# A second router written out phase by phase, and lookup tables with the columns innermost

## The reference, cut to what matters

```python
cap = N // E                       # 384
logits = x @ w_gate                # 3072 x 8
for idx in np.argsort(-logits.flatten()):
    tok, e = int(idx) // E, int(idx) % E
    if assigned[tok] >= 0 or counts[e] >= cap:
        continue
    assigned[tok] = e
    counts[e] += 1
for e in range(E):
    mask = assigned == e
    out[mask] = np.maximum(x[mask] @ w1[e], 0.0) @ w2[e]
```

## Time and profile before

| | us |
|---|---|
| median of 3 runs | 1102.71 |
| lowest, highest | 1101.93, 1104.84 |
| the profiled execution | 1102.15 |
| its span in the profile | 1100.1 |

### The profile page before, as it was taken

One profiled execution on the slowest core, in us unless ns is written; L12 is line 12 of the kernel. 1 busy time (PEld: TensorE's weight loads), 2 busy tenths in 40 slices (PEclk: granted clock), 3 DMA queues, 4 the chain that ended last, 5 costly groups with the idle time before them and its releaser, 6 DMA issues.

```text
span 1100.1 us, 22403 instructions
## 1 busy us (share of the span) xinstructions
PE 939.4 (85%) x6254; PEld 799.3 (73%) x6255; DVE 725.5 (66%) x1921; ACT 411.9 (37%) x885; POOL 189.9 (17%) x246
## 2 busy tenths in 40 slices
PE   7999999985599999999999973444379999999994
PEld 4888888874478888888888852333269898898984
DVE  5888888868865877868868685555735454555421
ACT  3555665545443452543534430000024343433410
POOL 1222222200111211111111110000021223312211
PEclk8999999998699999999999996555579999999997
DMA  9566666442161524515425150000034445354200
GB/s 217 128 145 143 141 146 145 96 154 108 54 243 38 191 63 176 191 48 199 139 100 183 48 191 31 0 0 0 1 90 151 166 150 210 123 185 156 89 29 29
DMA packets 146020, 129.13 MB, mean 117 GB/s; under 512 B 101936, under 2 KB 114224, under 8 KB 145840
## 3 DMA queue, kind: packets, MB, share of 16 engines
q1 hardware_dynamic: 137168, 99.67, 30.3%
q0 software_dynamic: 8800, 28.84, 7.7%
HBM read 107.78 MB, written 20.71 MB: 117 GB/s over the span
## 4 chain that ended last, share of the span: by engine, by line
PE 61%; DVE 17%; issue 9%; DVEq 5%; DMA 2%; ACTq 1%; ACT 1%; SPq 0%; POOL 0%; POOLq 0%
PE ps_o L1212 10%; PE ps_o L1585 8%; PE ps_s L1189 8%; PE ps_s L1569 6%; PE ps_pT L1569 6%; DVE product L1412 5%; PE ps_o L489 4%; PE ps_s L1585 4%; PE ps_t L1747 3%; PE ps_pT L470 3%; PE ps_s L457 3%; DVE arena_p L664 2%; PE ps_pT L1200 1%; DVEq L671 1%; DVEq L1415 1%
## 5 line engine op out<-in xcount | busy, mean ns | idle before, releaser
L1212 PE MATMUL ps_o<-w_split_parts,hs 128*128 x696 | 168.2, 398 | 10.7 <-ACT hs L1289 9.6
L1189 PE MATMUL ps_s<-w_split_parts,xs 128*128 x696 | 167.2, 396 | 1.5 <-ACT xs L1281 0.9
L1212 PEld LDWEIGHTS ps_o<-w_split_parts,hs 128*128 128x128 f32 x696 | 130.0, 190 | 38.6 <-issue 12.0
L1412 DVE SCALAR_TENSOR_TENSOR product<-y_sb,wg_all 128x512 bf16<-128x512 f32 x232 | 150.8, 687 | 6.8 <-ACT y_sb L1307 1.8
L1189 PEld LDWEIGHTS ps_s<-w_split_parts,xs 128*128 128x128 f32 x696 | 129.7, 190 | 28.0 <-issue 2.4
L773 ACT ACTIVATE arena_p<-arena_p,min_s 128x256 f32<-128x256 f32 (+1 forms) x192 | 91.7, 484 | 12.0 <-DVE min_s L653 10.9
L1585 PE MATMUL ps_o<-w_split_parts,hs 128*128 128x512 f32 x384 | 94.7, 398 | 0.0
L1403 DVE TENSOR_TENSOR w_split_parts<-raw,w_split_parts 128x1024 f32 (+1 forms) x68 | 78.7, 1220 | 5.9 <-ACT w_split_parts L1300 4.5
L1585 PEld LDWEIGHTS ps_o<-w_split_parts,hs 128*128 128x128 f32 x384 | 70.2, 188 | 16.5 <-ACT hs L1619 2.9
L1307 ACT ACTIVATE y_sb<-ps_o,gates 128x512 f32<-128x512 f32 x29 | 20.0, 689 | 164.9 <-DVE logits L1417 119.7
L1665 DVE TENSOR_TENSOR w_split_parts<-raw,w_split_parts 128x1024 fp32r<-128x1024 f32 x56 | 68.6, 1225 | 19.4 <-ACT w_split_parts L1627 19.0
(11 more groups left out here) (296 smaller groups left out, 1705.5 us busy)
## 6 DMA issues: line engine op xcount, KB each, us to landing
raw<-in_moe_w SPq DMA_DIRECT2D x32, 2048.0 KB, 9.8
y_rows<-y_sb POOLq DMA_DIRECT2D x31, 256.0 KB
kn<-in_k SPq DMA_DIRECT2D x32, 192.0 KB, 3.4
qn<-in_q SPq DMA_DIRECT2D x32, 192.0 KB, 3.5
vn<-in_v SPq DMA_DIRECT2D x32, 192.0 KB, 2.8
x_rows<-arena_x SPq DMA_DIRECT2D x96, 64.0 KB, 1.6
va<-in_v SPq DMA_DIRECT2D x32, 120.0 KB, 2.6
wg_rows<-in_moe_w_gate SPq DMA_DIRECT2D x1, 2048.0 KB, 7.7
```

The lines of the kernel that those rows point to most:

```text
L1189: last = nc.tensor.matmul(ps_s[:, f, :], xs[:, a, c * P:(c + 1) * P], weights(par, w, cols), start=(n == 0), stop=(n == len(passes) - 1))
L1212: last = nc.tensor.matmul(ps_o[:, 0, :], hs[:, a, c * P:(c + 1) * P], weights(par, 2 + w, slice(c * DM, (c + 1) * DM)), start=(n == 0), st ...
L1412: nc.vector.scalar_tensor_tensor(product[:, e % 2, :], y_sb[:], 1.0, wg_all[:, e, :], ALU.mult, ALU.mult, accum_out=log_now[:, e:e + 1])
```

## The change

Three parts, in the order of the diff.

**Tables.** One-hots and values get the column as the innermost index with a pitch of 32 (`COLS`), so every operand of the three DVE operations runs along columns. The numbers they are compared with are now full tensors, `block_no` (31 x 32) and `row_no` (128 x 32), made by POOL with two iotas (`number`) once after the attention's last transfers and turns and once again behind the first layer's experts, because the space is used for weights in between; DVE waits for them (`numbered`). Chunks are halves (12 and 12 columns, 16 and 15) in place of eights. PE's weights `row_hot[:, :, c]` and moving values `vals[:, :, c]` are read with a step of 32 elements.

**Phases.** All seven are written out on DVE and PE, without `apart` at three places. One subtraction and a minimum over the rooms at the end stand for the test in each phase, and `decided` is set there. The flag "expert has room" is replaced by the room itself times a large number, the copy of the rooms moves behind the compares of the next phase's first step, and the mark of the best expert moves behind the buckets. `CUTS` is 0, 8, 21, 31.

**POOL** waits for `decided` and branches before it waits for the tables.

```diff
-SHUT = 5.0e37
+SHUT = 5.0e34
+COLS = 32
...
         def chunks(cols):
-            cuts = list(range(0, cols, 8)) + [cols]
-            return [range(a, b) for a, b in zip(cuts, cuts[1:])]
+            half = cols // 4 * 2 if cols % 4 == 0 else (cols + 1) // 2
+            return [range(0, half), range(half, cols)]
+        def even(part):
+            return slice(part[0], part[0] + (len(part) + 1) // 2 * 2)
...
         def pe_table(pe, dst, seen, cols, sets, blocks):
-            vals = vals_of(cols, sets, blocks)
+            vals = vals_of(sets, blocks).rearrange("p s b c -> p (s b) c")
             for n, part in enumerate(chunks(cols)):
                 pe.wait_ge(row_hots, seen + n + 1)
                 for c in part:
-                    last = nc.tensor.matmul(dst[:, 0:sets * blocks], row_hot[:, c, :], vals[:, c].rearrange("p s b -> p (s b)"),
+                    last = nc.tensor.matmul(dst[:, 0:sets * blocks], row_hot[:, :, c], vals[:, :, c],
                                             start=(c == 0), stop=(c == cols - 1))
...
+        def dve_vals(part, sets, blocks, parts):
+            here = even(part)
+            shape = [P, sets, blocks, here.stop - here.start]
+            return nc.vector.tensor_tensor(vals_of(sets, blocks)[:, :, :, here],
+                                           hot[:, 0:blocks, here].unsqueeze(1).to_broadcast(shape),
+                                           parts[:, :, here].unsqueeze(2).to_broadcast(shape), ALU.mult)
...
         def dve_positions(dve, prods, cols, blocks, exact, parts, numbers, first=True):
+            nc.vector.memset(pos_r, 0.0)
+            nc.vector.memset(pos_b, 0.0)
             dve.wait_ge(r_p, prods)
...
                 nc.vector.tensor_scalar(e_a[0:1, 0:1], cumv[0:1, n - 1:n], float(NT), None, ALU.not_equal)
+                nc.vector.tensor_reduce(e_b[0:1, 0:1], room[0:1], AX, ALU.min)
...
-            if exact:
-                nc.vector.tensor_tensor(slow_f[0:1], slow_f[0:1], e_a[0:1, 0:1], ALU.max)
+            if exact and first:
+                nc.vector.scalar_tensor_tensor(slow_i[:], e_b[0:1, 0:1], 0.0, e_a[0:1, 0:1], ALU.is_lt, ALU.max).then_inc(decided, 1)
...
+            dve.wait_ge(numbered, numbers)
+            some = even(range(0, cols))
+            wide_hot = [P, blocks, some.stop]
+            nc.vector.tensor_tensor(hot[:, 0:blocks, some], block_no[:, 0:blocks, some],
+                                    pos_b[:, some].unsqueeze(1).to_broadcast(wide_hot), ALU.is_equal)
             for part in chunks(cols):
+                here = even(part)
+                done(nc.vector.tensor_tensor(row_hot[:, :, here], row_no[:, :, here],
+                                             pos_r[:, here].unsqueeze(1).to_broadcast([P, P, here.stop - here.start]), ALU.is_equal))
+                dve_vals(part, sets, blocks, parts).then_inc(row_hots, 1)
...
-            pool.wait_ge(tables, 3)
             pool.wait_ge(decided, 1)
             with pool.If(pool.value_load(slow_i[0:1, 0:1], min_val=0, max_val=1) > 0):
                 pool.wait_ge(slow_tables, 2)
+            pool.wait_ge(tables, 3)
             gather(0)
...
-        CUTS = (0, 5, 14, BLK1)
+        CUTS = (0, 8, 21, BLK1)
...
                         pe.wait_ge(rise_kept, ph + 1)
-                        apart(pe)
...
-            with pe.Fori(0, PHASES) as ph:
+            for ph in range(PHASES):
                 phase(ph)
...
-            def phase(ph, last):
+            def place(ph, last):
+                at = ph * FAST
                 dve.wait_ge(rise_made, ph + 1)
-                apart(dve)
                 nc.vector.scalar_tensor_tensor(rise, most.to_broadcast([WAYS, E]), 0.0, ps_pT[0:WAYS, 1, 0:E],
                                                ALU.is_ge, ALU.mult).then_inc(rise_open, 1)
                 dve.wait_ge(moved, at + FAST)
-                nc.vector.scalar_tensor_tensor(taken, bucket, th[:, 0:1], taken, ALU.is_ge, ALU.max)
+                nc.vector.tensor_scalar(taken, bucket, th[:, 0:1], 2.0 * SHUT, ALU.is_ge, ALU.mult)
                 dve.wait_ge(tallied, ph + 1)
-                apart(dve)
-                counts = ps_s[:, 2, 0:E]
-                done(nc.vector.tensor_tensor(room, room, counts, ALU.subtract))
-                done(nc.vector.tensor_scalar(e_a, room, 0.0, 2.0 * SHUT, ALU.is_gt, ALU.mult))
-                done(nc.vector.scalar_tensor_tensor(wide, col_b(taken, C), 2.0 * SHUT, exp_b(e_a, C), ALU.mult, ALU.add))
+                done(nc.vector.tensor_tensor(room, room, ps_s[:, 2, 0:E], ALU.subtract))
+                done(nc.vector.scalar_tensor_tensor(wide, exp_b(room, C), 2.0 * SHUT, col_b(taken, C), ALU.mult, ALU.add))
                 done(nc.vector.scalar_tensor_tensor(lw, wide, -SHUT, lw, ALU.add, ALU.min))
+                find_best(lw)
                 if last:
...
                 else:
-                    choose(lw)
+                    nc.vector.tensor_tensor(m_open, m, taken, ALU.add)
                     fill_buckets()
-                done(nc.vector.tensor_tensor_reduce(out=e_b[0:WAYS], in0=counts[0:WAYS], in1=room_open[0:WAYS], scale=1.0,
-                                                    scalar=-HUGE, op0=ALU.subtract, op1=ALU.max, accum_out=most))
-                nc.vector.scalar_tensor_tensor(slow_f[0:1], most[0:1], 0.0, slow_f[0:1], ALU.not_equal, ALU.max)
-                done(nc.vector.tensor_scalar(room_open, room, 1.0, None, ALU.max))
+                    nc.vector.tensor_tensor(hot_c, lw, col_b(m_open, C), ALU.is_equal)
+            def phase(ph):
+                at = ph * FAST
+                for j in range(FAST):
+                    search_step(at + j, j, bucket)
+                    if j == 0:
+                        if ph == 0:
+                            done(nc.vector.scalar_tensor_tensor(lw, col_b(left, C), span[:, 0:1], logits_2[:], ALU.mult, ALU.add))
+                        done(nc.vector.tensor_scalar(room_open, room, 1.0, None, ALU.max))
                     find_open(at + j, j, j == FAST - 1)
...
-            with dve.Fori(0, PHASES - 1) as ph:
-                phase(ph, False)
-            phase(PHASES - 1, True)
+            for ph in range(PHASES):
+                phase(ph)
...
+            def number():
+                g.iota(block_no[:], [[P, BLK1], [0, COLS]], base=0, **exact)
+                g.iota(row_no[:], [[1, P], [0, COLS]], base=0, **exact).then_inc(numbered, 1)
+            pool.wait_ge(lx_turned, TILES)
             pool.wait_ge(x_stored, 16 * PAIRS * QT)
+            number()
             pool_experts(pool)
+            number()
             pool_experts2(pool)
```

More of the change, by code:

```diff
@@ L105, in program @@
         code_e = sb("code_e", [P, E])
[L106 to L110, removed]
+        token_parts = sb("token_parts", [P, 2, COLS], bf16)
+        slot_parts = sb("slot_parts", [P, 4, COLS], bf16)
+        gate_parts = sb("gate_parts", [P, 3, COLS], bf16)
         first_th = sb("first_th", [P, WAYS])
@@ L994, in pe_table, with dve_positions @@
                 for c in part:
-                    last = nc.tensor.matmul(dst[:, 0:sets * blocks], row_hot[:, c, :], vals[:, c].rearrange("p s b -> p (s b)"),
+                    last = nc.tensor.matmul(dst[:, 0:sets * blocks], row_hot[:, :, c], vals[:, :, c],
                                             start=(c == 0), stop=(c == cols - 1))
             last.then_inc(tabled, 1)
[L999 to L1007, removed]
+        def dve_vals(part, sets, blocks, parts):
[4 more added lines that the diff above has]
+                                           parts[:, :, here].unsqueeze(2).to_broadcast(shape), ALU.mult)
+        def dve_positions(dve, prods, cols, blocks, exact, parts, numbers, first=True):
             def done(_):
@@ L1047, in dve_positions @@
             done(nc.vector.tensor_tensor(pos_b[:, 0:cols], pos[:, 0:cols], key_i[:, 0:cols], ALU.subtract))
[L1049 to L1052, removed]
-            for part in chunks(cols):
[L1054 to L1058, removed]
+            sets = parts.shape[1]
+            dve.wait_ge(numbered, numbers)
[3 more added lines that the diff above has]
+                                    pos_b[:, some].unsqueeze(1).to_broadcast(wide_hot), ALU.is_equal)
+            for part in chunks(cols):
+                here = even(part)
+                done(nc.vector.tensor_tensor(row_hot[:, :, here], row_no[:, :, here],
+                                             pos_r[:, here].unsqueeze(1).to_broadcast([P, P, here.stop - here.start]), ALU.is_equal))
+                dve_vals(part, sets, blocks, parts).then_inc(row_hots, 1)
         def dve_routing1(dve):
@@ L1113, in dve_routing1 @@
             for part in range(3):
-                done(nc.vector.tensor_copy(gate_parts[:, :, part], gate[:, 0:C]))
+                done(nc.vector.tensor_copy(gate_parts[:, part, 0:C], gate[:, 0:C]))
                 if part < 2:
```

(13 more changed lines are left out.)

89 lines of the change are left out of this document (43 added, 46 removed).

## The result

| | before | after |
|---|---|---|
| median of the runs | 1102.32 us (4 runs, 1101.9 to 1104.84) | 1090.11 us (4 runs, 1088.53 to 1092.57) |
| profiled execution, its span | 1102.15, 1100.1 | 1089.4, 1087.7 |

The ratio is 0.9887 (0.9862 to 0.9911): 12.2 us faster. The forecast was 17.2 us faster; the time lies in the stated range, 4.6 us above the forecast.

The account below looks back on a forecast made before the run. Both routers were taken as chains in which one engine works while the others wait. Terms for phases, POOL and tables summed to -17.2 us, from the median 1102.71 to 1085.5 us; own range 1083.5 to 1088, stated 1080.5 to 1093.

Parts of the forecast that it names:

- 1 compares recut: Search steps: compares cut at 8 and 21 let PE run on, 0.06 us for each of 28 steps, -1.7 us.
- 2 no `apart`: Phases: without the separate instructions behind waits, DVE and PE start sooner in each of 7 phases, -1.8 us.
- 3 phase's end: Phase's end on DVE: one step gone, -1.7; addition without drain, -1.1; test, rooms' copy and loop idle, -5.6 us.
- 4 first-time code: Written-out phases on DVE: code running for the first time stalls, 0 to 2.5 us, taken as +1.0.
- Rival C: Second router's start: DVE's scalar operations wait for the end of POOL's long iota, +2 us, 1087.5 us; chance 0.15.
- 7 second table: Second router's table: DVE at 0.52 ns an element, PE 0.13 us a pair, 7.1 against 10.21 us, -3.1.
- 7 first table: First router's table: faster DVE one-hots and values, then 12 matmuls, 4.8 against 7.28 us, -2.5.
- 7 gates' table: Gates' table: PE's 24 pairs cost +1.9 us, 1.14 falling into a wait, DVE's part 1.2 shorter; net 0.
- 6 POOL's copy: Behind the second table: POOL copies the first rows sooner, 0.86 us after it instead of 1.54, -0.7 us.
- Rival D: Written-out phases: first-time code stalls more, on DVE at every phase or PE in mid-count, +3 to +6, 1090 us; chance 0.11.
- rival A: Tables: DVE stays at one element a cycle, both token tables' gains gone, 1091.4 us; chance 0.12.
- Rival B: Tables on PE: strided load and values don't overlap, a pair takes 0.40 us, 1106.6 us; chance 0.05.

Follow-up runs that it names:

- experiment 6: Changed kernel with the compares cut at 5 and 14 again and three separate instructions (`apart`) back behind their waits in each phase: 1094.39 us, one run.
- experiment 2: Changed kernel with the tables as before (no iotas, chunks of 8); phases, exactness test and POOL's order as changed: 1088.79 us, ratio 0.9871.
- experiment 4: Changed kernel with columns innermost only in pairs, PE reading at a step of 2, small constants for the long iotas: 1082.0 us, ratio 0.9803.
- experiment 3: Changed kernel plus ten groups of 24 extra load-and-matmul pairs ahead of the second router, differing only in element step: 1107.09 us, one run.
- experiment 1: The changed kernel again, nothing altered, compared with the kernel before on the same chip: 1089.72 us, ratio 0.9873.
- experiment 5: Changed kernel with POOL's long iota (128 x 32) cut into 16 pieces, all else as changed: 1087.05 us, ratio 0.9849.

## Why the prediction was partly right

The sum, term by term, in us of the span; the measured column comes from the timelines and experiments above.

| step | forecast | measured | from |
|---|---|---|---|
| 1 compares recut | -1.7 | -2.2 | experiment 6, step 2.31 to 2.23 |
| 2 no `apart` | -1.8 | -2.2 | experiment 6, 7 x 0.31 |
| 3 phase's end | -8.4 | -8.6 | phase 14.20 before, 12.76 in experiment 6: 6 x 1.44 |
| 4 first-time code | +1.0 | -0.1 | stalls of 0.23 and 0.16, for the 0.50 of the earlier trace rows |
| 5 around the phases | 0 | -0.1 | start to compares 4.90 to 4.72 (experiment 2), last one-hot to table 4.82 to 4.90 |
| C DVE held by the iotas | 0 | +3.4 | router's start to compares 4.72 in experiment 2, 8.08 here |
| 7 second table | -3.1 | -1.6 | 10.21 to 8.57 |
| 7 first table | -2.5 | -2.0 | 7.28 to 5.26 |
| 7 gates' table | 0 | +1.1 | the rest of the -0.7 at the second router's start, with 0.2 of a later start of the first table |
| 6 POOL's copy | -0.7 | -0.9 | 1.54 to 0.67 behind the table |
| last layer | 0 | +0.8 | below |
| sum | -17.2 | -12.4 | spans -12.4 |

The gates' row is what remains of a difference and not a price of its own, and it holds for this one execution: in the four others with these tables the second router starts no earlier than before, which makes the row 1.9 to 2.5 there. The time lies in the stated range, 1080.5 to 1093, which was drawn to take in the rivals, but not in the forecast's own, 1083.5 to 1088. That it is no farther off is in part luck: the phases gave 2.3 us more than forecast, and without them the gain would have been 10, below the 12 that the prediction itself named as a sign of being wrong.

*The phases (1 to 4).* The mechanism was right and every term was a little small. From the first compares to the one-hot of the last phase it took 97.79 us and takes 84.62 (685.79 to 770.41), -13.2 for -10.9. The largest part of the difference is term 4: code that runs for the first time was expected to stall at two or more further places, and there are only two short stalls in all. Experiment 4's phases, which are the same code, had one of 0.44 (751.10) and took 0.5 longer, and experiment 2's had one of 0.47 (721.96), so it looks like chance and not like a fixed price; no run here decides it. Rival D was wrong in the other direction as well.

*DVE's side of the tables (7).* Right: 0.52 ns an element, and rival A is out in three kernels.

*PE's side of the tables (7).* This is the step that failed: "a pair takes 0.08 to 0.173, and I take 0.13". It takes 0.185, just outside the upper bound. The bound was the slope of DVE's reduction over a step of 124 bytes, 1.8 ns an element, and experiment 3 finds almost this number for PE, 1.8 to 2.0 ns a value. The middle was taken for no reason other than being the middle; the nearest row was the price itself. With 0.185 for 0.13 PE can't finish the first half under DVE's second, and becomes the bound of the table. The forecast's PE row to watch ("15 last matmuls in about 2.1 us") can't even be found: there is one unbroken group of 31. Rival B (a load and its matmul add up, 0.40 a pair) did not come: the values' read sets the pace, and the weights' adds little to it (groups with both steps 4.42 to 4.55 us at granted clocks of 0.60, 0.82 and 0.50, the values' step alone 4.09 at 1.00). Its time of 1106.6 also has a slip: the +7.3 for the gates' table leaves out the 1.22 us that the table took before.

*The gates' table (7).* "24 pairs at 0.13 each +1.9, of which 1.14 falls into PE's wait" became +3.0 (4.25 for 1.22) and a lower clock for the transposes behind (+0.8). The first 24 matmuls of the experts behind the first table are longer too, 7.70 us for 7.24 before, and 8.24 to 8.50 in the four other executions with these tables (7.19 and 7.30 in experiments 4 and 2, without them): in all five the clock comes back later, as in the last layer below. The prediction's own sign of failure, PE later at this place, did appear: up(1) starts at 301.35 against 299.44 in the span. Later waits absorbed a part.

*Rival C.* Given 0.15 and +2, it happened and cost 3.4. The argument against it, "no DVE row beside POOL's work is longer than its kind", was an argument from absence: none of these rows stood beside a long instruction of POOL. The price was also too small, because the iota starts 1.84 us behind the last transfer and DVE's operation met nearly all of its 4.17. *The Trainium skill (SBUF — State Buffer, "Who interferes with whom") says that `tensor_scalar` may take both ports and that the one that comes second waits for the other's whole instruction; the runs agree: 3.88 us beside an iota of 4.17, 0.22 beside sixteen of 0.33 each (5.25 / 16).*

*The last layer.* From its first split matmuls to the end of the span before took 292.36 us (1100.1 - 807.74), the changed kernel 293.17, and its first 24 matmuls 7.16 us for 6.25. The windows of these matmuls, of the kernel before and of the changed one (columns as above, the granted clock is third from the end):

```profile
807.74:814.00 6.26, 6.26 (x25) 6.26 (x26) 1.14 (x2) 1.44 (x2) 2.14 (x3) 0.68 0.43 126
```

```profile
794.53:801.70 7.17, 7.17 (x25) 7.17 (x26) 1.78 (x2) 1.43 (x2) 2.14 (x3) 0.58 0.39 110
```

The clock comes back later. The five executions with values read at a step of 64 bytes all have it: the first 24 matmuls take 7.16, 7.24, 7.21, 7.17 and 6.75 us (here and in experiments 1, 3, 5 and 6), the rest of the span is 293.17, 293.31, 292.95, 292.92 and 292.79. The three without it don't: 6.25, 6.25 and 6.37, and 292.36 before, 292.32 in experiment 2, 292.47 in experiment 4. That the strided table does it was not tried by itself, so the cause is open.

So the gain that is missing went to four places: 3.4 us to POOL's iota, 2.0 us to PE in the two token tables, 1.1 to the gates' table and 0.8 to the last layer, while the phases gave 2.3 more. Experiment 4 takes all four back. By the spans it is 6.4 us under the changed kernel: 1.4 until the second router starts, 3.4 in its start, 1.8 in the table and 0.7 in the last layer, less 0.5 in its phases and 0.35 between POOL's copy and the first split matmul.

## What to carry to other kernels

When a layout is turned for the engine that bounds a stage, cost it for every engine that reads the same tile: here one engine got its elements at twice the rate, the next reader took more than twice as long over them (0.185 us a pair for 0.08), and pairs of two gave both what they need. Where a price is unknown between two bounds and one of them is a measured row of the same kind of access, take that row and not the middle. A long instruction put on an engine "because it is idle" is free only if no small operation of its neighbour falls under it; look at which one stands in its window, or cut it up.

## What the runs showed of the hardware that was not expected

- bf16 values at a step of 16 to 64 bytes cost TensorE 1.8 to 2.0 ns each, with little regard to the granted clock (24 x 96 in 4.09 us at 1.00, 4.55 at 0.50) and to the step's size. A step of 8 bytes in both operands already costs: 0.092 us a pair at a granted clock of 0.65, for 0.079 adjacent at 0.50. A step of 4 bytes in both doesn't: 2.10 us for 24 pairs at 0.50, as adjacent (2.08).
- Weights at a step of 64 bytes cost much less than values: 0.063 us a pair at a granted clock of 1.00, for 0.044 with adjacent ones.
- VectorE keeps the doubled rate on bf16 when only the two innermost elements are adjacent and all outer indices repeat: 2048 in 1.22 us in experiment 4, as in the changed kernel; with the repeated index innermost 1.22 us were 1024 elements.
- A 2x2 operation on VectorE was held for 3.66 us (3.88 less its 0.22) by an iota that reads nothing; in 16 pieces the same iota did not hold it.
- A separate instruction behind a wait cost DVE 0.12 us (0.15 against 0.03).
